# New orders in the lone attention, and the end of a batch: two remainders of x on GpSimd, x waited for tile by tile

## The reference, cut to what matters

```python
scores = q @ k.T / sqrt(64), causal          # per head
local = softmax(scores) @ v
q_p = phi(q)                                 # where(q > 0, q, exp(q) - 1) + 1
mem_out = (q_p @ M_prev) / (q_p @ z_prev + 1e-6)
x = g * mem_out + (1 - g) * local            # g = sigmoid(beta), per head
x = (sigmoid(x @ w_gate) * (x @ w_val)) @ w_out       # 512 -> 1536 -> 512
h = x @ w_in                                          # 512 -> 2048
out = (h * clip(h + 3, 0, 6) / 6) @ w_out2            # 2048 -> 512
```

## Time and profile before

| | us |
|---|---|
| three runs | 1123.38, 1124.30, 1125.17 |
| median of the runs | 1124.3 |
| the profiled execution | 1123.45 |
| span of its instructions | 1121.6 |

### The profile page before, as it was taken

The page is one execution under the profiler, slowest core; times in us unless marked ns, Lnnn a source line. Parts: engine busy times, 40 slices in busy tenths (PEclk is TensorE's granted clock), DMA queues, the critical chain, the costliest instruction groups (busy, mean ns, idle before and its releaser), DMA issues.

```text
span 1121.6 us, 21910 instructions
## 1 busy us (share of the span) xinstructions
PE 1091.8 (97%) x6928; PEld 1015.0 (90%) x6928; DVE 582.7 (52%) x1314; ACT 559.3 (50%) x1258; POOL 499.7 (45%) x517
## 2 busy tenths in 40 slices
PE   4998999999999999999999999999999999999998
PEld 3667999998999999999999999998999999899997
DVE  5888757767757757766733333723323232232322
ACT  4776676676775776776754333223323232232322
POOL 5889657656767656666543444993000000000000
PEclk9999999999999999999999999999999999999999
DMA  7551542442443443343222232440000000000000
GB/s 181 132 128 37 131 111 71 121 110 63 104 115 83 110 111 81 101 114 89 75 68 68 85 84 84 117 129 29 28 0 28 0 28 0 0 28 0 29 1 29
DMA packets 100229, 81.41 MB, mean 73 GB/s; under 512 B 7760, under 2 KB 85584, under 8 KB 100176
## 3 DMA queue, kind: packets, MB, share of 16 engines
q1 hardware_dynamic: 100176, 80.77, 27.0%
HBM read 76.03 MB, written 4.72 MB: 72 GB/s over the span
## 4 chain that ended last, share of the span: by engine, by line
PE 87%; DVE 4%; issue 3%; POOL 2%; DMA 1%; ACT 1%; DVEq 0%; SPq 0%; POOLq 0%; ACTq 0%
PE ps L604 82%; PE ps L645 4%; PE ps L659 1%; POOL prob L531 1%; DMA stage<-w_gate 1%; DVE prob L1233 1%; DVE phi L1215 1%; DVE x_lo L1248 1%; DMA stage<-w_val 0%; POOL WO L518 0%; ACT pt_hi L931 0%; ACT prob L976 0%; DVE znorm_e L1205 0%; DVE znorm L1203 0%; ACT L976 0%
## 5 line engine op out<-in xcount | busy, mean ns | idle before, releaser
L604 PE MATMUL ps<-x_hi,WG 128*128 128x288 f32 x1536 | 324.4, 297 | 4.3 <-DVE pt_lo L1181 2.5
L604 PEld LDWEIGHTS ps<-x_hi,WG 128*128 128x128 f32 x1536 | 251.3, 188 | 7.3 <-DVE pt_lo L1181 2.9
L604 PE MATMUL ps<-x_lo,WG 128*128 128x288 f32 x768 | 226.1, 294 | 0.0
L604 PE MATMUL ps<-c_hi,W 128*128 128x384 f32 x768 | 210.3, 337 | 0.0
L518 POOL TENSOR_TENSOR WG<-stage,WG 128x512 fp32r<-128x512 f32 x96 | 129.8, 1368 | 119.6 <-ACT WG L959 119.6
L604 PE MATMUL ps<-W,g_hi 128*128 128x512 f32 x576 | 179.0, 391 | 0.0
L1397 DVE SCALAR_TENSOR_TENSOR g_raw<-g_raw,ps 128x384 f32<-128x384 f32 x96 | 53.2, 554 | 221.0 <-ACT g_raw L1122 220.8
L604 PE MATMUL ps<-h_hi,WO 128*128 128x288 f32 x768 | 164.6, 297 | 0.4 <-DVE Y L1379 0.2
L1122 ACT ACTIVATE g_raw<-ps 128x384 f32<-128x384 f32 x96 | 47.3, 492 | 215.3 <-PE ps L604 215.3
L531 POOL TENSOR_SCALAR prob<-prob,rscale 128x128 f32<-128x128 f32 (+4 forms) x160 | 108.7, 697 | 83.8 <-DVE rscale L1193 83.8
L604 PEld LDWEIGHTS ps<-x_lo,WG 128*128 128x128 f32 x768 | 144.2, 188 | 0.5
(11 more groups left out here) (106 smaller groups left out, 1849.3 us busy)
## 6 DMA issues: line engine op xcount, KB each, us to landing
stage<-w_out SPq DMA_DIRECT2D x64, 256.0 KB, 2.7
qk_st<-qk_t SPq DMA_DIRECT2D x54, 288.0 KB, 4.3
stage<-w_gate SPq DMA_DIRECT2D x48, 256.0 KB, 3.4
stage<-w_val SPq DMA_DIRECT2D x48, 256.0 KB, 3.1
qn_st<-q_n SPq DMA_DIRECT2D x16, 256.0 KB, 3.1
stage<-w_in SPq DMA_DIRECT2D x16, 256.0 KB, 2.7
out<-y_out SPq DMA_DIRECT2D x5, 768.0 KB, 3.6
v_st<-v_n SPq DMA_DIRECT2D x12, 256.0 KB, 2.7
```

What stands on the lines that cost most here:

```text
L604: return pe.matmul(o, l, r, start=start, stop=stop, skip_group_check=True)
```

## The change

Eight edits. The order of work in each engine's list changes; what is computed does not.

1. SyncE: V and M of pair 0 and the first three weight blocks are no longer loaded ahead of `walk`, but in `lead`: V and M behind the load of q and k for head 2, the blocks behind that for head 3. The weight blocks of the lone attention are split one head later each (`first_block`).
2. TensorE, p = 1 of all five pairs: `turn_phi(n, 0)` goes behind scores of tile 3 and behind the products with V.
3. VectorE, p = 1: `row_scales` goes ahead of `phi_scaled`; in pair 0 the mask of tile 1 goes ahead of `phi_scales`.
4. ScalarE, p = 1: the move of phi goes behind exp of tile 2 and behind x_high; for pair FIRST x_high, M and head tiles change places (on VectorE too, with x_rest and low_m).
5. Y isn't zeroed. The first quarter of a batch (q = 0) copies its PSUM tile into Y; the others add. For this the loops over q start at 1, the round q = 0 is written out, and the loop over b is written out as a Python loop.
6. Batch end: x_lo of tiles 1 and 2 is made by GpSimd, between two of the weight splits of p = 1, slots 1 and 3. VectorE makes tile 0 in slot 2 as before, tile 3 behind unit O6 and its moved tile, ahead of O7.
7. TensorE waits for x_lo before each tile's products of G0, and not for all four ahead of them.
8. VectorE makes the remainders of M (`low_m`) behind the output units O4 and O5, not ahead of them.

```diff
-        LOW_X = {2: (0,), 3: (1, 2), 4: (3,)}
+        LOW_X = {2: (0,), 4: (3,)}
+        MIDDLE_X, OUTER_X = (1, 2), (0, 3)
...
         def first_block(n, p):
-            k = 2 * n + p - 1
+            k = 2 * n + p - 2
...
-            with eng.Fori(0, whole) as b:
-                with eng.Fori(0, QPB - 1) as q:
+            for b in range(whole):
+                pair(b * QPB + LAG, b * QPB, b, 0)
+                with eng.Fori(1, QPB - 1) as q:
                     pair(b * QPB + q + LAG, b * QPB + q, b, q)
...
-            with eng.Fori(0, r - 1 - whole * QPB) as q:
+            pair(whole * QPB + LAG, whole * QPB, whole, 0)
+            with eng.Fori(1, r - 1 - whole * QPB) as q:
...
-            with eng.Fori(0, QPB - 1) as q:
+            quarter(n_pairs - QPB, 0)
+            with eng.Fori(1, QPB - 1) as q:
...
                 load_qk(u + 2)
+                if u == 0:
+                    for j in two:
+                        load_m_first(0, j)
+                    load_tiles(v_first[0], v_n, 0, ld_v_first[0])
+                if u == 1:
+                    for k in range(NST):
+                        stage_block(0, 0, k)
...
-            stage_block(0, 0, 0)
-            load_tiles(v_first[0], v_n, 0, ld_v_first[0])
-            for j in two:
-                load_m_first(0, j)
-            for k in range(1, NST):
-                stage_block(0, 0, k)
...
-            def low_ws(r, p):
-                for slot in CUT[p]:
+            def middle_x(b):
+                for k in MIDDLE_X:
+                    pool.wait_ge(xc_hi, DT * b + k + 1)
+                    pool.tensor_tensor(x_lo[:, k, :], x_new[:, k, :], x_hi[:, k, :].bitcast(F32), ALU.subtract).then_inc(xc_lo_mid, 1)
+
+            def low_ws(r, p, cut):
+                for i, slot in enumerate(CUT[p]):
+                    if cut is not None and p == 1 and i == 2:
+                        middle_x(cut)
...
-                for x, at in enumerate(ZERO_Y):
-                    if (n, p) == at:
-                        pool.memset(Y[:, :, x * S:(x + 1) * S], 0.0).then_inc(y_zero, 1)
...
-                if t == 0:
-                    pe.wait_ge(xc_lo, DT * (b + 1))
...
                 for k in range(DT):
+                    if t == 0 and k in MIDDLE_X:
+                        pe.wait_ge(xc_lo_mid, len(MIDDLE_X) * b + MIDDLE_X.index(k) + 1)
+                    elif t == 0:
+                        pe.wait_ge(xc_lo, len(OUTER_X) * b + OUTER_X.index(k) + 1)
...
                     v_tiles(0)
                     v_tiles(1)
-                    turn_phi(n, 0, None)
                     scores(n, p, 3)
                     v_tiles(2)
                     v_tiles(3, 4)
+                    turn_phi(n, 0, None)
                     turned_tile(0)
...
                     cut_q(n + 1, 0)
-                    move_phi(n, 0)
                     exp_tile(n, p, 2)
                     if old:
                         x_high(n - 1, 1)
+                    move_phi(n, 0)
                     move_tile(n, 0, 0)
...
+                    exp_tile(n, p, 2)
                     move_hi(n, p, "phi", 0, None)
-                    exp_tile(n, p, 2)
-                    x_high(n - 1, 1)
                     move_hi(n, p, "head", 0, None)
                     move_hi(n, p, "phi", 1, None)
+                    move_hi(n, p, "head", 1, None)
+                    x_high(n - 1, 1)
                     exp_tile(n, p, 3)
...
                     mask_tile(n, 1, 0)
+                    if n == 0:
+                        mask_tile(n, 1, 1)
                     phi_scales(n)
                 elif n < FIRST:
-                    mask_tile(n, p, 1)
+                    if n >= 1:
+                        mask_tile(n, p, 1)
+                    row_scales(n, p)
                     phi_scaled(n)
-                    row_scales(n, p)
...
                     move_lo(n, p, "phi", 0, None)
-                    x_rest(n - 1, 1)
                     move_lo(n, p, "head", 0, None)
                     move_lo(n, p, "phi", 1, None)
+                    move_lo(n, p, "head", 1, None)
+                    x_rest(n - 1, 1)
                     mask_tile(n, p, 4)
...
-                    if p == 1 and turn and i == 3:
-                        low_m(n)
-                    if cut is not None and p == 1 and i == QT - 1:
-                        cut_x(cut, LOW_X[i])
...
-                            dve.tensor_tensor(y, ps[:, out_bank(j, alone), 0:HALF], y, ALU.add).then_inc(f_y, 1)
+                            if isinstance(q, int) and q == 0:
+                                dve.tensor_copy(y, ps[:, out_bank(j, alone), 0:HALF]).then_inc(f_y, 1)
+                            else:
+                                dve.tensor_tensor(y, ps[:, out_bank(j, alone), 0:HALF], y, ALU.add).then_inc(f_y, 1)
                             if j >= OU - 2:
                                 moves(i, slice(j - (OU - 2), j - (OU - 2) + 1))
+                            if cut is not None and j == OU - 2:
+                                cut_x(cut, LOW_X[i])
+                    if p == 1 and turn and i == 3:
+                        low_m(n)
```

More of the change, by code:

```diff
@@ L186, in attention_and_mlps @@
         ld_qk, ld_v, ld_phi, ld_m, ld_beta = [sem(x) for x in ("ld_qk", "ld_v", "ld_phi", "ld_m", "ld_beta")]
-        init, y_zero, m_zero = sem("init"), sem("y_zero"), sem("m_zero")
+        init, m_zero = sem("init"), sem("m_zero")
         g_e, g_1, g_r, gates = sem("g_e"), sem("g_1"), sem("g_r"), sem("gates")
@@ L201, in attention_and_mlps @@
         w_hi, w_done = sem("w_hi"), sem("w_done")
-        xc_hi, xc_lo = sem("xc_hi"), sem("xc_lo")
+        xc_hi, xc_lo, xc_lo_mid = sem("xc_hi"), sem("xc_lo"), sem("xc_lo_mid")
         f_gate, f_val, f_gout, f_vout = [sem(x) for x in ("f_gate", "f_val", "f_gout", "f_vout")]
@@ L271, in attention_and_mlps @@
                ((), ((1, 2), (1, 3)), (), ((1, 4), (1, 5)), ()))
-        ZERO_Y = ((3, 1), (4, 0), (4, 1), (4, 1))
         def walk(eng, lead, step):
@@ L471, in _ @@
                          (ld_v, 2 * DMA * FIRST), (v_hi_done, 2 * FIRST), (v_ready, 2 * FIRST),
-                         (ld_m, DMA * FIRST), (m_hi_done, 2 * FIRST), (m_ready, 2 * FIRST), (xc_hi, DT), (xc_lo, DT)):
+                         (ld_m, DMA * FIRST), (m_hi_done, 2 * FIRST), (m_ready, 2 * FIRST), (xc_hi, DT),
+                         (xc_lo, DT - len(MIDDLE_X)), (xc_lo_mid, len(MIDDLE_X))):
                 pool.sem_inc(s, c)
@@ L571, in step @@
                     phi_by_z(n)
-                low_ws(r, p)
+                low_ws(r, p, cut)
             wait_qk(0)
@@ L1045, in lead @@
                     cut_q(n + 1, 0)
+                    exp_tile(n, p, 2)
                     move_hi(n, p, "phi", 0, None)
-                    exp_tile(n, p, 2)
-                    x_high(n - 1, 1)
                     move_hi(n, p, "head", 0, None)
                     move_hi(n, p, "phi", 1, None)
+                    move_hi(n, p, "head", 1, None)
+                    x_high(n - 1, 1)
                     exp_tile(n, p, 3)
-                    move_hi(n, p, "head", 1, None)
+                    move_hi(n, p, "head", 2, None)
+                    move_hi(n, p, "head", 3, None)
                     act.wait_ge(m_zero, 2)
                     high_m(n)
-                    move_hi(n, p, "head", 2, None)
                     exp_tile(n, p, 4)
-                    move_hi(n, p, "head", 3, None)
             def step(n, p, old, turn, scoring, r, b, q, cut):
@@ L1110, in chunk2 @@
                     act.wait_ge(f_val, GV * n_pairs + 1)
-                    act.wait_ge(xc_lo, DT * B)
                     act.wait_ge(f_y, OU * (QPB + 1))
@@ L1305, in lead @@
                     move_lo(n, p, "phi", 0, None)
-                    x_rest(n - 1, 1)
                     move_lo(n, p, "head", 0, None)
                     move_lo(n, p, "phi", 1, None)
+                    move_lo(n, p, "head", 1, None)
+                    x_rest(n - 1, 1)
                     mask_tile(n, p, 4)
-                    move_lo(n, p, "head", 1, None)
-                    low_m(n)
                     move_lo(n, p, "head", 2, None)
                     move_lo(n, p, "head", 3, None)
+                    low_m(n)
             def cut_chunk(n):
@@ L1370, in step @@
                             j = int(unit[1])
-                            if j == 0:
-                                if not has_next_quarter(r):
-                                    cut_chunk(0)
-                                dve.wait_ge(y_zero, B)
+                            if j == 0 and not has_next_quarter(r):
+                                cut_chunk(0)
                             y = Y[:, j // 2, bass.ds(b * S + (j % 2) * HALF, HALF)]
```

1 line of the change is left out of this document (removed).

## The result

| | before | after |
|---|---|---|
| median, us | 1124.3 (1123.38 to 1125.17) | 1111.1 (1110.06 to 1112.64) |
| the profiled execution, its span | 1123.45, 1121.6 | 1112.64, 1110.8 |

The ratio is 0.988, 95% interval 0.987 to 0.990: 13.2 us by the medians, 10.8 between the two profiled executions. The forecast was 1112.7. The executions of this kernel lay up to 2.6 us apart, and the profiled one is the slowest of them; a second set of four had the median 1111.2 (ratio 0.989, 0.987 to 0.990).

The account below looks back on a forecast made before the run. TensorE, busy 97% of the span, was taken to bound the kernel, so only its waits could be won. Terms 2.8 + 1.9 + 2.0 + 0.9 + 2 x 1.25 + 0.5 + 1.05 = 11.65 us gave 1112.7, range 1108.5 to 1118.5.

Parts of the forecast that it names:

- ceiling of 16.0: Whole kernel: TensorE's waits apart from the start, 16.0 us, taken as the most the change could win.
- the phi row: Sign, TensorE's waits for phi: their total was to fall from 6.8 us to under 1.5.
- Pairs 0 and 1: Start of the lone attention: shorter waits for phi and the first scaled tile, 2.8 us off pair 0, 0.9 off pair 1.
- Pairs 2 to 4: Rest of the lone attention: shorter waits for phi and moves, 0.9 us off pair 2, 0.1 pair 3, 2.0 pair 4.
- The h_val wait of quarter 0: Quarter 0: TensorE's 0.69 us wait, laid to Y's zeroing holding up a small VectorE operation; 0.6 us off.
- The loop over b: Jump back of this loop: writing it out removes TensorE's wait behind VectorE's 2.68 us stand; 1.05 us off.
- code reading: Rival, six written-out pieces: code first read stalls engines as the jump did, up to 16.1 us, 1128.8; chance 0.06.
- Batch ends 1 and 2: TensorE's 1.24 us wait ahead of G0 goes as VectorE's way to Y and `pt_lo` shortens; 1.25 us each off.
- The shared port: Rival, batch ends: GpSimd's two remainders hold VectorE up, the waits stay; 3.0 us less gain, 1115.7; chance 0.07.
- End 3: Batch end 3: TensorE's waits of 0.2 and 0.53 us for Y shrink; 0.5 us off.
- VectorE is what comes next in the lone attention: Rival, lone attention: VectorE holds it and new orders only move waits; 3.9 us less gain, 1116.6; chance 0.16.
- Every wait goes: Rival, whole kernel: the ceiling but for 0.5 us is won, 1108.8 or lower; chance 0.07.

Follow-up runs that it names:

- after_zeroed: The changed kernel with Y zeroed on GpSimd and added to in every quarter, as before the change: 1113.6 us, ratio 0.991.
- after_straight: The changed kernel with the loops over q written out as well, no jump left in the attention: 1111.3 us, ratio 0.989.
- after_middle_dve: The changed kernel with x_lo of tiles 1 and 2 on VectorE again, at its old place: 1112.9 us, ratio 0.990.
- attention_only: The kernel before with only the new orders of the lone attention (edits 1 to 4): 1120.4 us against 1123.9, ratio 0.997.
- loops_only: The kernel before with b and the round q = 0 written out, Y still zeroed and added to: 1122.2 us against 1123.9, ratio 0.998.
- bloop_only: The kernel before with only the loop over b written out, loops over q and zeroing kept: 1123.8 us against 1124.1, ratio 1.000.
- batch_end_only: The kernel before with only the new batch end (edits 6 to 8): 1122.5 us against 1123.9, ratio 0.999.
- after_warm: The changed kernel with 15 unused transposes on TensorE ahead of the first scores and 12 ahead of pair 0's phi: 1109.0 us, ratio 0.986.

## Why the prediction was right, and where it was not

The forecast is 1.6 us above the median, and its mechanism is the right one: TensorE's waits in the first 100 us and at the batch ends. Of 11.65 us in the sum 10.8 came between the two profiled executions, 12.1 in the second one of the kernel after, 13.2 between the medians. That the sum lies so near is in part luck: pairs 0 and 1 brought 1.3 to 2.7 us less than said, and quarter 0, the loop over b and batch ends 1 and 2 together about 2 us more. The ceiling of 16.0 should have been 16.9, since 0.9 for masks was left out, and the terms' own bounds add up to 3.4 to 15.9 and not to 8 to 15. Of the signs, two were missed: the phi row fell to 2.5 and not under 1.5, and a pair takes 17.3 us and not 17 or less. Point by point:

**Pairs 0 and 1: 3.7 said, 1.05 seen in the first profile, 2.4 in the second.** The waits went as said: phi is turned at 19.03 (said 18.8), the first scaled tile at 19.94 and not 22.46. TensorE's standing ahead of pair 2 fell from 15.56 us to 11.90, and to 12.57 in the second execution, which is 3.66 and 3.0. But for the same 139 products it was busy for 2.6 us longer, and 0.6 in the second execution (before, then after, from the start to pair 2; columns as in rows 3):

```profile
0.00:45.06 45.06, 29.50 (x139) 21.36 (x140) 30.11 (x79) 26.85 (x69) 29.84 (x49) 1.00 0.66 160
0.00:44.01 44.01, 32.11 (x139) 23.26 (x140) 29.59 (x81) 26.23 (x67) 28.72 (x48) 1.00 0.65 156
```

What the sum left out is TensorE's clock. The column of the granted clock has no record ahead of the first change and prints 1.00 there, so I read it from the products. Four of 288 columns, in the kernel after, ahead of 28.5 us and behind it:

```profile
21.32 0.44 PE L613 MATMUL ps<-k_lo,q_s 128*128 128x288 f32 x1
21.56 0.44 PE L613 MATMUL ps<-k_hi,q_s 128*128 128x288 f32 x1
...
30.74 0.29 PE L613 MATMUL ps<-k_hi,q_s 128*128 128x288 f32 x1
30.87 0.29 PE L613 MATMUL ps<-k_lo,q_s 128*128 128x288 f32 x1
```

They start 0.24 us apart, then 0.13: 1.2 and 2.4 GHz. The record begins where the spacing changes: at 25.8 us before, at 28.5 in the first execution after and at 24.3 in the second. Those 4.2 us between the two stand beside 1.3 us in the time of pair 2: about 0.3 us for each. Three more kernels with the same pairs 0 and 1 (after_zeroed, after_straight, after_middle_dve) fit: the record begins at 23.5, 23.9 and 24.7, and pair 2 comes at 42.27, 42.62 and 42.85. The term was sized on waits alone; with the clock as in before it would have been about 1.9, by my estimate from these 0.3. So even then half of it would be missing: while the clock is at 1.2 GHz, work that moves into a wait that is gone takes twice as long as it would have behind 25.8 us. Why the moment differs between executions of one kernel is open.

**Pairs 2 to 4: 3.0 said, 2.67 seen.** Single pairs, from phi to phi: 18.00, 17.18 and 18.66 before, 17.26, 17.36 and 17.28 after. Pair 3 lost 0.2 where 0.1 of gain was said, but not for the reason given, that a weight remainder of GpSimd would stretch phi_scaled: it took 0.81 there, and 0.82 in the pairs around it. Pair 2, pair 3, then pair 4 of the kernel before:

```profile
55.99 0.82 DVE L1225 TENSOR_TENSOR phi<-phi,zscale 128x640 f32<-128x640 f32 x1
73.36 0.81 DVE L1225 TENSOR_TENSOR phi<-phi,zscale 128x640 f32<-128x640 f32 x1
```

```profile
91.36 1.88 DVE L1215 TENSOR_TENSOR phi<-phi,zscale 128x640 f32<-128x640 f32 x1
```

So the new orders also gave VectorE 0.8 us in pairs 1 and 2, where the earlier trace rows had 1.61, and 1.06 in pair 4. "17 us or less" was not reached, since TensorE now waits 0.25 to 0.26 for a mask and 0.31 for a move in pairs 2 and 3, 0.57 together; pair 3 had only 0.38 to lose, for phi, and that is its 0.2. Of the 2.67, 1.22 are the orders (attention_only) and 1.5 the zeroing: I had given most to the orders.

**The h_val wait of quarter 0: a step that was half right.** It was laid to a VectorE operation held up by the zeroing of Y, like the one in the earlier trace rows. loops_only keeps the zeroing and has no such wait, attention_only keeps zeroing, loops and wait. It comes from a weight block that ScalarE has to wait for; both the zeroing and the entry of the loop over q with a register make it late, and the written-out round alone removes the wait: 1.15 and not 0.6.

**The loop over b: too small.** Said 1.05 and 0.3, measured 2.0 for the jump (bloop_only) and 2.18 with the written-out round. I took the wait next to the jump from the earlier trace rows and 0.3 of h_val's 0.51. The quarter's waits were 1.64 together, and TensorE's busy time in it, which no view of waits shows, fell by another 0.55 (42.09 to 41.54). Of code reading nothing was seen, and the rival of it is refuted by after_straight. The Trainium skill says that a taken jump to code outside the current window stalls until it is fetched ("Runtime: NRT & Kernel Launch", section "Instruction fetch mechanics"); the 2.68 and 3.14 us on VectorE at the jump over two pairs, and none in straight code, agree; that the time is spent on fetching, no run shows.

**Batch ends 1 and 2: 1.25 each said, 1.5 measured.** GpSimd paid next to nothing, as said: TensorE waited 0.23 for a weight remainder at end 2. The shared port did show, at a place I had not looked: `low_m`, moved behind O4 and O5, now runs beside GpSimd's second remainder and the weight remainder behind it and took 2.04 us for its two and not 0.46. In after_middle_dve, without the remainders on GpSimd, they took 0.43. VectorE had the room. By the Trainium skill ("SBUF — State Buffer", section "Who interferes with whom") two-input operations there shut each other out; this row agrees. **End 3:** 0.5 said, 0.2 to 0.5 seen.

**The parts do not add up.** Alone they won 3.5, 1.4 and 1.7, 6.6 us of 13. Of the missing 6.4, the batch end and the loop over b together win 3.3 more than apart: without the other, the one gives 1.03 back at the jump, and the other loses 0.50 to a longer wait at batch end 2 and 1.35 to the lower clock behind it. The intervals of the three ratios leave the 3.3 uncertain by some 2.6; in the profiled executions, from quarter 1 to the end, the two won 5.12 together and 2.24 and 0.57 alone, 2.3 more. Another 2.5 is the zeroing, which can only go once the round q = 0 is code of its own. The rest, 0.6, is less than these medians can tell.

**The rivals.** VectorE is what comes next in the lone attention, but it did not take the gain. "Every wait goes" is not so far off: TensorE's waits behind the first product fell from 16.9 to some 7, of which 2.45 are pair 0's phi.

## What to carry to other kernels

Try two repairs on one path together before you drop either: here a wait removed in one place came back at the next jump, and the parts alone showed half of the whole. Try writing out the first round of a short loop where its entry feeds a DMA ring, and keep long loop bodies from jumping back in the middle of a tight chain. Where a trace begins with a lone, gappy stretch, read the spacing of equal products in it, and count the products at the lower clock as well as the waits; idle products in the gaps can be worth it (2.1 us here).

## What the runs showed of the hardware that I had not expected

- TensorE's clock came to its full level for good at 18.9 to 31.6 us of the span, by kernel and by execution: 25.8 before, 28.5 and 24.3 in two executions after, 31.6 with the batch end alone, which changes nothing in that stretch, 18.9 with idle transposes. In three of the traces it had been full before, for 3.4 to 6.8 us, and had fallen again.
- It can drop again in full work: behind waits of 1.67 and 1.74 us it was at 1.2 GHz for 3.3 to 3.4 us in two kernels; behind one of 2.10 at the jump, in the profiled execution of batch_end_only, it was not. Nine of that kernel's ten executions have a mean granted clock under 1, the profiled one has 1.000, so it may have dropped in others. What tells these apart is open.
- Two small operations of VectorE on 64 x 64 values took 2.04 us and not 0.46 beside two-input operations of GpSimd, and one on 128 x 10 values 1.16 beside GpSimd's k_lo. In after_warm that operation took 0.17, and the delay fell on a later one of the same size (1.00).
